# Attention, then two feed-forward stages, on one core: another order of the first three attention steps on TensorE, ScalarE and GpSimd

## What is computed

```
def phi(x):
    proj = np.einsum('bhsd,df->bhsf', x, w_phi)
    proj = proj - np.max(np.abs(proj), axis=-1, keepdims=True)
    return np.concatenate([np.exp(proj), np.exp(-proj)], axis=-1)
q_p, k_p = (phi(q), phi(k))
kv = np.einsum('bhsf,bhsd->bhfd', k_p, v)
z = np.sum(k_p, axis=2)
num = np.einsum('bhsf,bhfd->bhsd', q_p, kv)
den = np.einsum('bhsf,bhf->bhs', q_p, z)[..., None] + 1e-06
return (num / den).astype(np.float32)
```

## Time and profile before

| | |
|---|---|
| median of 3 runs | 867.81 us (866.08 to 868.11) |
| the profiled execution, its own time | 865.15 us |
| its span | 863.3 us |
| TensorE busy in the span | 841.3 us (97%) |
| VectorE, ScalarE, GpSimd busy | 403.6, 340.8, 243.0 us |
| TensorE busy from 0 to 10 us | 6.83 us |
| TensorE busy from 100 to 150 us | 49.03 us |

### The profile page before, as it was taken

The page is one execution under the profiler, slowest core; times in us unless marked ns, Lnnn a source line. Parts: engine busy times, 40 slices in busy tenths (PEclk is TensorE's granted clock), DMA queues, the critical chain, the costliest instruction groups (busy, mean ns, idle before and its releaser), DMA issues.

```text
span 863.3 us, 19447 instructions
## 1 busy us (share of the span) xinstructions
PE 841.3 (97%) x7168; PEld 727.6 (84%) x7169; DVE 403.6 (47%) x730; ACT 340.8 (39%) x751; POOL 243.0 (28%) x286
## 2 busy tenths in 40 slices
PE   7999999799999999999999999999999999999996
PEld 5999999599899899789988889998778888888885
DVE  5677778321255345425535664552872442432221
ACT  4676777311146226315603522541432432532221
POOL 5877877694000000000000000029251121212111
PEclk9999999999999999999999999999999999999999
DMA  7553443049321012101201111514441341311111
GB/s 183 129 140 106 120 135 76 26 147 26 2 85 62 25 49 61 37 1 74 70 6 55 57 36 41 202 39 154 150 143 55 129 146 36 128 49 43 36 37 43
DMA packets 36088, 67.68 MB, mean 78 GB/s; under 512 B 11336, under 2 KB 11464, under 8 KB 36040
## 3 DMA queue, kind: packets, MB, share of 16 engines
q1 hardware_dynamic: 26168, 44.90, 19.5%
q10 hardware_dynamic: 6512, 11.64, 4.3%
q0 software_dynamic: 3360, 10.49, 3.7%
HBM read 57.58 MB, written 9.98 MB: 78 GB/s over the span
## 4 chain that ended last, share of the span: by engine, by line
PE 89%; POOL 3%; DVE 3%; ACT 2%; issue 1%; DMA 1%; ACTq 0%; POOLq 0%; DVEq 0%
PE bank L1681 23%; PE bank L1683 23%; PE bank L1682 23%; PE bank L1626 4%; PE bank L1571 3%; PE bank L1596 3%; PE bank L1870 2%; PE bank L1581 1%; PE bank L1733 1%; PE bank L1822 1%; PE bank L1612 1%; PE bank L1752 1%; PE bank L1559 1%; DVE stage L1159 1%; ACT stage L983 1%
## 5 line engine op out<-in xcount | busy, mean ns | idle before, releaser
L1128 DVE SCALAR_TENSOR_TENSOR hid_lo<-bank,hid_hi 128x384 fp32r<-128x384 f32 x96 | 53.5, 557 | 210.5 <-ACT hid_hi L959 210.5
L1681 PE MATMUL bank<-uT_hi,W 128*128 128x384 f32 x384 | 129.4, 337 | 0.3 <-DVE uT_lo L1147 0.3
L1683 PE MATMUL bank<-uT_hi,W 128*128 128x384 f32 x384 | 129.5, 337 | 0.0
L1682 PE MATMUL bank<-uT_lo,W 128*128 128x384 f32 x384 | 128.9, 336 | 0.0
L959 ACT ACTIVATE hid_hi<-bank 128x384 fp32r<-128x384 f32 x96 | 46.9, 488 | 184.9 <-PE bank L1683 184.8
L983 ACT ACTIVATE stage<-stage 128x512 f32<-128x512 f32 x135 | 84.6, 627 | 79.2 <-DVE stage L1159 72.7
L1681 PE MATMUL bank<-W,hid_hi 128*128 128x512 f32 x288 | 114.1, 396 | 0.6 <-DVE hid_lo L1128 0.6
L1683 PE MATMUL bank<-W,hid_lo 128*128 128x512 f32 x288 | 113.6, 395 | 0.0
L1682 PE MATMUL bank<-W,hid_hi 128*128 128x512 f32 x288 | 113.4, 394 | 0.0
L1159 DVE TENSOR_TENSOR stage<-rows,stage 128x512 f32<-128x512 f32 x135 | 89.0, 687 | 10.4 <-ACT stage L983 8.5
L1390 DVE TENSOR_TENSOR hT_lo<-bank,hT_hi 128x512 fp32r<-128x512 f32 x40 | 27.6, 691 | 105.3 <-ACT hT_hi L1020 105.3
(11 more groups left out here) (287 smaller groups left out, 1526.4 us busy)
## 6 DMA issues: line engine op xcount, KB each, us to landing
rows<-in_moe_w SPq DMA_DIRECT2D x12, 1024.0 KB, 6.0
stage<-gate_rows ACTq DMA_DIRECT2D x38, 256.0 KB, 3.3
stage<-in_moe_w_ch SPq DMA_DIRECT2D x16, 512.0 KB, 4.1
qk_raw<-in_q SPq DMA_DIRECT2D x32, 144.0 KB, 3.4
vv<-in_v SPq DMA_DIRECT2D x32, 144.0 KB, 2.8
x_rows<-rows SPq DMA_DIRECT2D x6, 768.0 KB, 3.2
qk_raw<-in_k SPq DMA_DIRECT2D x30, 144.0 KB, 3.4
late_stage<-in_moe_w SPq DMA_DIRECT2D x4, 1024.0 KB
```

Of the source, the lines that this page charges most:

```text
L1128: dve.scalar_tensor_tensor(out=hid_lo[:, n % 2], in0=bank[:, HB[n % 2], 0:TOK], scalar=0.0, in1=hid_hi[:, n % 2].bitcast(F32), op0=ALU.max ...
L1681: pe.matmul(dst, lhs_hi, rhs_hi, start=start, stop=False)
L1682: pe.matmul(dst, lhs_hi, rhs_lo, start=False, stop=False)
L1683: return pe.matmul(dst, lhs_lo, rhs_hi, start=False, stop=stop)
```

## The change

In steps 0 to 2 TensorE's list is written out anew; from step 3 on it is as before. Step 0 turns only the first group. Step 1 projects that group, turns the second, and from there on projections and turns alternate. The `keep_busy` product between the groups of step 0 is gone. In step 2 the first 24 of the 36 state products come ahead of the turns of unit 2, and the key sums (split off as `sum_up`) come after the second turns. On ScalarE `exp_k(0, par, 1)` comes ahead of `exp_q(0)` in step 2. On GpSimd one `place_v` moves behind `sum_keys(0)`, and each `rest_of_v` moves behind the next unit's `sum_keys`.

```diff
-            for n in range(3):
+            for n in range(2):
                 place_v(n)
             sum_keys(0)
             pool.wait_ge(k_summed, 1)
-            place_v(3)
+            for n in range(2, 4):
+                place_v(n)
             round_v()
-            rest_of_v(0)
             sum_keys(1)
             pool.wait_ge(k_summed, 2)
-            rest_of_v(1)
+            rest_of_v(0)
             for u in range(2, UNITS):
                 sum_keys(u)
+                if u == 2:
+                    pool.wait_ge(k_summed, 3)
+                    rest_of_v(1)
...
-                    exp_q(0)
                     if is_step(s, 2):
                         exp_k(0, par, 1)
+                    exp_q(0)
                     exp_k(s - 2, par, 2)
...
                 def transposes(s, par, g):
-                    if is_first(s) and g == 1:
-                        keep_busy(1, 1)
+                    if is_step(s, 0) and g == 1:
                         pe.wait_ge(qk_loaded[0], 32)
...
-                def state():
+                def state(ts=range(T)):
                     u = s - 2
-                    pe.wait_ge(v_loaded[par], 32 * (u // 2) + 32)
-                    if not (isinstance(u, int) and u == 0):
-                        pe.wait_ge(n_out, OUTS * u)
-                    for t in range(T):
+                    if 0 in ts:
+                        pe.wait_ge(v_loaded[par], 32 * (u // 2) + 32)
+                        if not (isinstance(u, int) and u == 0):
+                            pe.wait_ge(n_out, OUTS * u)
+                    for t in ts:
...
+                if is_step(s, 0):
+                    first_turn()
+                elif is_step(s, 1):
+                    pe.wait_ge(const_loaded, 32)
+                    project(0)
+                    pe.wait_ge(t_out, 1)
+                    transposes(0, 0, 1)
+                    project(1)
+                    first_turn()
+                    project(2)
+                    second_turn()
+                elif is_step(s, 2):
+                    project(0)
+                    q_turn(0)
+                    project(1)
+                    state(range(2 * GT))
+                    first_turn()
+                    state(range(2 * GT, T))
+                    q_turn(1)
+                    project(2)
+                    turn_kv()
+                    second_turn()
+                    sum_up()
```

More of the change, by code:

```diff
@@ L1597, in state @@
                                                kp[par][rr, t // GT, t % GT, sign, :], start=(t == 0), stop=(t == T - 1))
-                    mm.then_inc(kv_done, 1)
+                    if T - 1 in ts:
+                        mm.then_inc(kv_done, 1)
                 def turn_kv():
@@ L1607, in turn_kv, with sum_up @@
                                          ident[rr, rr])
+                def sum_up():
+                    u = s - 2
                     pe.wait_ge(k_summed, u + 1)
@@ L1628, in output, with first_turn @@
                     mm.then_inc(n_done, 1)
[L1630 to L1641, removed]
+                def first_turn():
                     if is_first(s):
@@ L1650, in step, with second_turn @@
                     transposes(s, par, 0)
[L1651 to L1664, removed]
+                def second_turn():
                     if older:
@@ L1669, in step, with q_turn @@
                     transposes(s, par, 1)
+                def q_turn(g):
+                    if g == 1 and newest:
+                        pe.wait_ge(t_out, NT * s + 1)
+                    elif g == 0 and newer:
+                        pe.wait_ge(t_out, NT * s)
+                    else:
+                        pe.wait_ge(qp_done, OUTS * (s - 2) + g)
+                    turn_q(g)
+                if is_step(s, 0):
[21 more added lines that the diff above has]
+                    sum_up()
+                else:
+                    if older:
+                        q_turn(0)
+                    if newer:
+                        project(0)
+                        project(1)
+                    if newest:
+                        first_turn()
+                    if older:
+                        state()
+                        if is_step(s, UNITS + 1):
+                            side(first_jobs[1], 1)
+                        q_turn(1)
+                    if newer:
+                        project(2)
+                    if older:
+                        turn_kv()
+                        sum_up()
+                    if newest:
+                        second_turn()
                 if older:
```

## The result

| | before | after |
|---|---|---|
| median, 17 runs each on the same chip | 866.88 us (865.42 to 868.11) | 868.84 us (865.86 to 870.61) |
| ratio of after to before | | 1.002, 95% interval 1.001 to 1.0029 |
| profiled execution, its own time and span | 865.15 and 863.3 us | 865.86 and 864.0 us |

In these runs the changed kernel was 2 us slower, where 1.45 us less had been forecast, and the median lies just outside the forecast range. By the bound of 0.3% it still reads as no change; the interval of the ratio says that it is a loss. The profiled execution of the changed kernel happens to be the shortest of its 17, so its trace shows less than the whole loss. The profile of e5 stands nearer to the median.

A forecast was written before the change was run, and what follows sets the result against it. GpSimd's chain from 15.41 to 31.30 us was taken as the early bound, before TensorE, busy nearly throughout, sets the pace. -2.70 + 1.25 = -1.45 us from a median of 867.81 gave 866.4 us, range 864.0 to 868.6.

The forecast's parts named there:

- Part 1: GpSimd between units 0 and 1: L751 leaves the chain (-2.70 us), one copy of V enters (+1.25), net -1.45 us.
- Part 2: Start of GpSimd's chain, L762 of unit 0: later projection and earlier key exponentials cancel, 15.4 us as before, within 0.05.
- Part 3: TensorE in step 2: no time won or lost, sums at 20.5, output at 21.6; moved loads cost nothing.
- Part 4: TensorE before unit 1's sums: at full clock ready by 29.7 us, GpSimd later at 29.99, so the gain is 1.45.
- Part 5: GpSimd between units 2 and 3: the second L751's 2.64 us fit 2.68 us of idle time; otherwise some 0.1 us lost.
- The sum: Whole kernel: early gains carry to the end as a shift, -1.45 us, giving 863.7 us profiled and 866.4 us median.
- B: Start, some 8.3 to 11.7 us: half clock after idle time delays GpSimd's chain 1.0 us; 867.4 us, chance 0.20.
- C: Start: half clock from before the first projection past the second, L762 1.75 us late; 868.1 or 869.4 us, chance 0.12.
- D: Unit 0's output: only the clock's fall at 22 us comes again, leaving 0.2 us gain; 867.6 us, chance 0.11.
- E: GpSimd's idle-time fit or late third exponentials holding L768: another wait takes the gain back; 867.8 us, chance 0.07.

The follow-up runs named there:

- e5: The changed kernel again, word for word, for another profile and more times: 868.12 us, ratio 1.0003 to before.
- e3: The changed kernel with one filler product put back ahead of the first projection: 869.11 us.
- e10: The changed kernel with four filler products after the first turns and both first `w_ch1` pieces loaded behind unit 4's queries and keys: 867.22 us.
- e2: The kernel before without its filler product between the two groups of turns in step 0: 867.23 us, ratio 1.0007.
- e4: The changed kernel with the first two `w_ch1` pieces (1 MB) loaded behind unit 4's queries and keys instead of ahead: 867.69 us, ratio 1.0008.
- e8: The changed kernel with GpSimd's order of before: 866.48 us.
- e15: The changed kernel with one of the first two `w_ch1` pieces left in place and the other (0.5 MB) behind unit 5's loads: 866.5 us, ratio 0.9999.
- e11: The kernel before with only the first two `w_ch1` pieces moved behind unit 4's queries and keys: 867.84 us.
- e13: The changed kernel with TensorE's old steps 0 and 1, filler included, and the second `w_ch1` piece behind unit 5's loads: 865.64 us, ratio 0.9979.
- e14: The changed kernel with four filler products after the first turns and the second `w_ch1` piece behind unit 5's loads: 865.34 us, ratio 0.9974.
- e6: The changed kernel with TensorE's steps 0 and 1 as before, filler included: 867.31 us.

## Why the prediction was wrong, step by step

- **Part 1 (GpSimd's net 1.45 us): right.** From the start of L762 in unit 0 to the end of unit 1's `k_sum` are 14.48 us in the changed kernel (16.27 to 30.75), and in before 15.41 to 31.31, which is 15.90; the difference is 1.42.
- **Part 2 (the chain begins at 15.4): wrong by 0.86 us in the changed kernel,** because projections and turns at 0.50 stretched the start. In e3 and e10, with fillers and a full clock, L762 (L763 in e10) starts at 15.32 and 15.42. The working of the part was right for a full clock; the clock itself was the open question.
- **Part 3 (output at 21.6): 22.55,** 0.95 late for the same reason; 21.59 in e3, 21.70 in e10. The output took 2.32 us as forecast.
- **Part 4 ("Does TensorE follow?"): the step that failed.** It counted TensorE's work, not whether its instructions are there. By its sum the sums stood at 29.99; they started at 31.89. Of the 1.90 us, 0.86 (with rounding 0.89) are GpSimd's late start. GpSimd was ready for TensorE at about 30.88 (30.75 and the 0.13 between 31.31 and 31.44 in the earlier trace rows), and the remaining 1.01 us is the wait of 1.35 less 0.34 that TensorE would have waited for GpSimd anyway. In e10, without both, they start at 30.08. The sum closes: -1.45 + 0.86 + 1.01 is 0.42, and unit 1's output came 0.41 us later than in the earlier trace rows.
- **Part 3 again, "I cost them at nothing":** I asked of the loads only when their data is needed, not what else uses the queues between 24 and 28 us. Unit 4's loads did not go out earlier (21.54 us, and 21.52 before). The values went 1.61 us later (19.29 and 17.68), not 0.5, and with them the `w_ch1` pieces behind them, which the part doesn't name. That is the other half of the same miss.
- **Part 5 (L751 just fits): right.** The second L751 ends and L695 follows 0.19 us later, and no wait of TensorE for `k_sum` stands behind it.
- **The sum, "most is carried to the end as a shift":** the profiled execution lost 0.41 us at unit 1's output and 0.7 in the span. The typical loss is larger, since the fetch wait varies (1.35 and 2.46 in two profiles of one kernel) and the clock can fall behind it (e5).
- **The rivals.** B and C had the mechanism of the clock right: it fell at 8.4, for 6.8 us, longer than B's and with other places than C's. Its price on the path, 0.86, was just below B's 1.0 and half of C's 1.75. The rule of the Trainium skill, TensorE: Matmul & The Clock Gate, "The HAM clock gate", that recent activity is what releases the half clock, agrees as far as single profiles go: the clock fell between 8 and 13 us in the changed kernel, e2, e4, e5, e8 and e15, all without the filler, and of those with one only in e11. D did not come in either profile of the changed kernel. E was the right kind of case, a wait that takes the gain back, but its two candidates were not the one, and it was priced at no change and not as a loss.

What stays open: no row names the issue waits as fetches; that they are rests on the packets' times in 18 profiles, on the fixed place in the list and on their going with the load (e4, e13 to e15). How much of the two extra microseconds of the first 17 runs is this wait, and how much is the clock in other places (between 152 and 177 us in eight profiles), was not separated, and the second measurement (e5) has only a third of the loss. That e8 has the better median, by 1.6 us beside e5 in the same batch, is not explained beyond this.

## What to carry to other kernels

Before an engine is made to come earlier to a stretch of code that runs once, or a bulk load later, look at the DMA load at that moment: besides data, its own instructions travel there. A bulk load with slack should go out when the engine is in a loop, or in pieces between the others. Taking it apart brought the changed kernel level with before (e15), and together with fillers, or with the old steps 0 and 1, about 2 us below it (e14, e13). And when a bound is lifted, list what it had been hiding: in e2 and e8 the same wait cost nothing.

## What the runs showed of the hardware

- TensorE waited 0.28 to 2.46 us between 26 and 28 us, each time until 1.26 to 1.52 us after a 16 KB packet of the instruction queue had landed. That packet took 0.96 to 1.45 us itself; what the load added was the delay of its start, up to 3.8 us.
- The hardware loop needs none: in the kernel before no q8 packet starts between 53 and 150 us, where four start between 28 and 45 us.
- In e3 TensorE waited 4.62 us at 228 us for no semaphore. The q8 packet before it started at 223.8 us and took 5.8 us; in the kernel before and the changed one the packet of that stretch started at 206.7 and 210.8. That this is the same kind of wait is likely, not shown, as TensorE went on 3.3 us after the packet's end. From 216 to 226 us of e3 the queues held 851 packets with next to no bytes, and were busy for more than half the time:

```profile
q1 hardware_dynamic: 851, 0.00, 55.5%
q8 instruction: 1, 0.02, 3.6%
```

- The half clock can follow such a wait, which then costs more than itself: 2.46 us of idle time in e5 made unit 1's output 2.2 us later than 1.35 us did. It doesn't always: behind 2.38 us in e10 and 1.86 us in e6 the clock stayed at 1.00.
- The slow start is not in the clock's row: in e14 twelve products took 1.65 us before 10 us, as at 0.50, where the windows read 1.00. The trace's own record of the clock begins only at 10.8 us there. In the six profiles with a slow start it begins at 10.4 to 13.8 us, in the other twelve at 4.6 to 6.4, so the windows read 1.00 where there is no record.

```profile
8.37 1.65 PE L1574 MATMUL bank<-wphi,qkT 64*128 64x128 f32 x12
```

```profile
8.00:9.00 1.00, 1.00 (x9) 0.78 (x9) 0.00 (x0) 0.00 (x0) 0.00 (x0) 1.00 1.02 221
```
